# The first weights' products of two MLP layers by Strassen's seven half products, on one Trainium2 core

## The reference, cut to what matters

```python
# attention: x is (1152, 512)
h = np.maximum(x @ w_in, 0.0)                 # w_in 512 x 2048
x = h * h @ w_out                             # w_out 2048 x 512
p = domain_probs / (domain_probs.sum(-1, keepdims=True) + 1e-09)
for e in range(4):                            # w1[e] 512 x 1024, w2[e] 1024 x 512
    out += p[:, e:e + 1] * (np.maximum(x @ w1[e], 0.0) @ w2[e])
```

## Time and profile before

| | |
|---|---|
| device time, three runs | 663.77, 667.1, 667.3 us; median 667.1 |
| the profiled execution's own time | 664.17 us |
| its span | 662.4 us |
| mean granted PE clock | 0.997 of full |
| busy: PE, DVE, ACT, POOL | 641.6, 233.4, 152.7, 201.0 us |
| DMA | 35.51 MB, mean 54 GB/s |

### The profile page before, as it was taken

How to read it: one execution, slowest core, us unless ns; L and a number is a source line. 1 busy time by engine, 2 the same in 40 slices (tenths; PEclk the granted TensorE clock), 3 DMA queues, 4 the chain that set the end, 5 groups by cost and what they waited for, 6 DMA issues and landing times.

```text
span 662.4 us, 9433 instructions
## 1 busy us (share of the span) xinstructions
PE 641.6 (97%) x3684; PEld 601.5 (91%) x3684; DVE 233.4 (35%) x580; ACT 152.7 (23%) x377; POOL 201.0 (30%) x138
## 2 busy tenths in 40 slices
PE   6968999999999999999999999999999999999997
PEld 5858899999999999989898989898989898989896
DVE  5895945152956262312121212121212121212121
ACT  3776302031302031402031402031402031302020
POOL 4575725065915067500005500004500004500000
PEclk9999999999999999999999999999999999999999
DMA  8451300004310004310004210003300004010101
GB/s 323 162 172 62 96 33 0 1 1 128 94 34 1 1 0 128 97 33 0 1 1 127 95 32 0 0 0 127 95 32 0 0 0 127 0 48 0 48 0 48
DMA packets 16075, 35.51 MB, mean 54 GB/s; under 512 B 2480, under 2 KB 2736, under 8 KB 16048
## 3 DMA queue, kind: packets, MB, share of 16 engines
q1 hardware_dynamic: 16048, 35.15, 16.5%
HBM read 32.79 MB, written 2.36 MB: 53 GB/s over the span
## 4 chain that ended last, share of the span: by engine, by line
PE 91%; DVE 6%; DMA 1%; issue 1%; SPq 0%; POOL 0%; DVEq 0%; ACT 0%
PE ps L664 29%; PE ps L665 29%; PE ps L666 29%; DVE y_acc L460 1%; DVE probT_buf L485 1%; DMA raw<-in_moe_w_in 1%; PE ps L614 1%; PE ps L653 1%; PE ps L661 1%; DVE h_lo L509 1%; DVE h_hi L505 1%; PE ps L634 1%; DVE x_lo L491 0%; DVE wa_hi L498 0%; DVE ssum L476 0%
## 5 line engine op out<-in xcount | busy, mean ns | idle before, releaser
L664 PE MATMUL ps<-x_hi,wa_hi 128*128 128x384 f32 x576 | 193.2, 335 | 0.2 <-DVE h_lo L509 0.2
L666 PE MATMUL ps<-x_hi,wa_lo 128*128 128x384 f32 x576 | 192.6, 334 | 0.0
L665 PE MATMUL ps<-x_lo,wa_hi 128*128 128x384 f32 x576 | 192.5, 334 | 0.0
L442 ACT ACTIVATE h_hi<-ps 128x384 fp32r<-128x384 f32 x96 | 47.2, 492 | 318.8 <-PE ps L666 318.8
L313 POOL TENSOR_TENSOR wa_lo<-raw,wa_hi 128x1024 fp32r<-128x1024 f32 x24 | 57.1, 2404 | 202.9 <-ACT wa_hi L394 197.3
L666 PE MATMUL ps<-wb_hi,h_lo 128*128 128x512 f32 x288 | 112.3, 390 | 0.0
L665 PE MATMUL ps<-wb_lo,h_hi 128*128 128x512 f32 x288 | 112.3, 390 | 0.0
L664 PE MATMUL ps<-wb_hi,h_hi 128*128 128x512 f32 x288 | 112.0, 389 | 0.0
L664 PEld LDWEIGHTS ps<-x_hi,wa_hi 128*128 128x128 f32 x576 | 108.2, 188 | 1.1 <-DVE h_lo L509 0.5
L665 PEld LDWEIGHTS ps<-x_lo,wa_hi 128*128 128x128 f32 x576 | 108.2, 188 | 0.4
L666 PEld LDWEIGHTS ps<-x_hi,wa_lo 128*128 128x128 f32 x576 | 108.1, 188 | 0.0
(11 more groups left out here) (58 smaller groups left out, 494.3 us busy)
## 6 DMA issues: line engine op xcount, KB each, us to landing
raw<-in_moe_w SPq DMA_DIRECT2D x32, 512.0 KB, 3.6
raw<-in_moe_w_in SPq DMA_DIRECT2D x8, 512.0 KB, 5.1
raw<-in_moe_w_out SPq DMA_DIRECT2D x8, 512.0 KB, 4.2
out_acc<-in_q SPq DMA_DIRECT2D x8, 288.0 KB, 4.4
out_acc<-in_k SPq DMA_DIRECT2D x8, 288.0 KB, 4.4
result<-out_acc SPq DMA_DIRECT2D x8, 256.0 KB, 2.0
hid_tmp<-in_v_near SPq DMA_DIRECT2D x4, 384.0 KB, 4.5
v_str<-in_v_far SPq DMA_DIRECT2D x4, 320.0 KB, 6.1
```

The lines of the kernel that those rows point to most:

```text
L442: nc.scalar.activation(h_hi[:, ft, :], ps[:, ABANKS[ft % NB], 0:CH], ACT.Relu)\
L664: nc.tensor.matmul(dst, a_hi, b_hi, start=first, stop=False)
L665: nc.tensor.matmul(dst, a_hi, b_lo, start=False, stop=False)
L666: return nc.tensor.matmul(dst, a_lo, b_hi, start=False, stop=last)
```

## The change

The product of the first weights (`w_in`, `w1`) with the activations is no longer made tile by tile. Weights of a group of 512 features (k x f = 512 x 512) are cut into four quarters A11 to A22, the activations of a chunk of 576 tokens into four quarters B11 to B22 (halves of k, halves of 288 tokens). Seven products M1 to M7 of half size, of sums of quarters (S1 to S4, T1 to T4), and sums of these products (in Winograd's order: second, third, fourth sum, C11, C22, C21, C12) give the block's four quarters of hidden activations. The seven operand forms of each side are split into high and low as before. The parts:

- Groups of 512 features: 4 in the first layer and 2 for each of the 4 experts, 12 in all (`SUBS`), x 2 chunks of 576 tokens = 24 blocks `t`. PE's order is A0, A1, B0, A2, B1, ... A7, B6, B7, A8, A9, B8, ... (`A`: the seven products of a block, `B`: its outputs). All engines run it unrolled.
- Every product is 2 tiles (`u`) of 2 k-tiles x 3 passes of 288 columns. Products use banks in pairs: X (M1, M2, M4), Y (M6, M7, M3), Z (M5). Outputs use two banks in turn: in the first layer 8 tiles a block of 4 x 3 passes of 288 columns, in the experts 5 tiles for even and 4 for odd blocks, of 4 x 3 passes of 512 columns. An output tile waits for the DVE sum (`y_tile`, `out_tile`) of the tile two before.
- ACT copies M1 to SBUF (`first_product`), casts all forms (`wa_high`, `x_high`, `wb_high`) and hidden activations (`h_high`). POOL makes the low parts of all weight forms and x forms and the weights' sums S1 to S4 (`sums`; those of group 0 are DVE's), and no squares any more. DVE makes the T forms, all sums of products, the squares in place (`square`, one operation with ReLU), `h_low` from SBUF, and the outputs' sums.
- Attention's result goes to `y` (`att_out`, ACT), not to `x_hi` and `x_lo`; forms of chunk 0 are made in pairs 4 to 7 of the attention, those of chunk 1 behind it, those for the experts around B6, B7 and A8.
- Weights are laid out on the host in the order of the blocks; a group's first weights come as 4 DMAs of 256 KB, its second as 2 of 512 KB.

The core of the diff; `out_tile` is like `y_tile` with L592's operation on 512 columns. `t_forms` and `x_high` wait for the attention's or the first layer's results.

```diff
-    FT = F // P
-    CHUNKS = 3
-    CH = N // CHUNKS
-    TT = CH // P
-    PIECES = 4
-    NB = 4
-    UNITS = CHUNKS * FT
-    SPLIT_WITH = {0: [0, 1], 3: [2], 4: [3]}
+    GF = 512
+    FT = GF // P
+    MOE1_SUBS = 4
+    EXPERT_SUBS = 2
+    SUBS = MOE1_SUBS + EXPERTS * EXPERT_SUBS
+    CT = N // 2
+    HT = CT // 2
+    FORMS = 7
+    A11, S2, A12, S3, S1, A22, S4 = range(FORMS)
+    B11, T2, B21, T3, T1, T4, B22 = range(FORMS)
+    M1, M6, M2, M7, M5, M4, M3 = range(FORMS)
+    X, Y, Z = 2, 4, 0
+    PRODUCT_BANK = [X, Y, X, Y, Z, X, Y]
+    BBANK = 6
+    C11, C22, C21, C12 = range(4)
+    EVEN_TILES = 5
+    TILES = N // P
+
     LOCAL_CONSTANTS = 7
     CONSTANTS = LOCAL_CONSTANTS + 3
...
+        BLOCKS1 = 2 * MOE1_SUBS
+        ORDER = [("A", 0)]
+        for t in range(1, BLOCKS1):
+            ORDER += [("A", t), ("B", t - 1)]
+        ORDER += [("B", BLOCKS1 - 1), ("A", BLOCKS1)]
+        for t in range(BLOCKS1 + 1, 2 * SUBS):
+            ORDER += [("A", t), ("B", t - 1)]
+        ORDER += [("B", 2 * SUBS - 1)]
...
+            def wa_low(s, k):
+                where, i = {A11: (raw_a, 0), A12: (raw_a, 1), A22: (raw_a, 3),
+                            S1: (s_form, 0), S2: (s_form, 1), S3: (s_form, 2), S4: (s_form, 3)}[k]
+                pool.wait_ge(s_wa_hi, FORMS * s + k + 1)
+                nc.gpsimd.tensor_tensor(wa_lo[:, k, :, :], where[:, i, :, :], wa_hi[:, k, :, :].bitcast(F32),
+                                        ALU.subtract).then_inc(s_wa_lo, 1)
...
+            def sums(s):
+                pool.wait_ge(s_raw_a, 64 * (s + 1))
+                pool.wait_ge(s_wa_hi, FORMS * s)
+                pool.wait_ge(s_wa_lo, FORMS * s)
+                nc.gpsimd.tensor_tensor(s_form[:, 0, :, :], raw_a[:, 2, :, :], raw_a[:, 3, :, :], ALU.add)\
+                    .then_inc(s_s, 1)
+                nc.gpsimd.tensor_tensor(s_form[:, 2, :, :], raw_a[:, 0, :, :], raw_a[:, 2, :, :], ALU.subtract)\
+                    .then_inc(s_s, 1)
+                pool.wait_ge(s_s, 4 * s + 1)
+                nc.gpsimd.tensor_tensor(s_form[:, 1, :, :], s_form[:, 0, :, :], raw_a[:, 0, :, :], ALU.subtract)\
+                    .then_inc(s_s, 1)
+                pool.wait_ge(s_s, 4 * s + 3)
+                nc.gpsimd.tensor_tensor(s_form[:, 3, :, :], raw_a[:, 1, :, :], s_form[:, 1, :, :], ALU.subtract)\
+                    .then_inc(s_s, 1)
...
+            def x_low(i, k):
+                c = i % 2
+                pool.wait_ge(s_xf_hi, FORMS * i + k + 1)
+                if k == T2:
+                    pool.wait_ge(s_t, 4 * i + 3)
+                if i == 1 and k == 0:
+                    pool.wait_ge(s_pv, NP - 2)
+                src = x_blocks(c)[0].get(k, t_form[:, c, k, :, :])
+                nc.gpsimd.tensor_tensor(xf_lo[:, c, k, :, :], src, xf_hi[:, c, k, :, :].bitcast(F32),
+                                        ALU.subtract).then_inc(s_xf_lo, 1)
...
+            for k in range(FORMS):
+                x_low(1, k)
+            for kind, t in ORDER:
+                s = t // 2
+                if kind == "A" and t % 2 == 0 and s + 1 < SUBS:
+                    sums(s + 1)
+                if kind == "A" and t % 2 == 1:
+                    for d in range(KT):
+                        wb_low(s, d)
+                    if s + 1 < SUBS:
+                        for k in range(FORMS):
+                            wa_low(s + 1, k)
+                if kind == "B" and t in (BLOCKS1 - 2, BLOCKS1 - 1):
+                    for k in range(FORMS):
+                        x_low(t - BLOCKS1 + 4, k)
 
...
+            def first_product(t):
+                for u in range(2):
+                    act.wait_ge(s_m, products(t, M1, u))
+                    if t > 0:
+                        act.wait_ge(s_c, 8 * (t - 1) + u + 1)
+                    nc.scalar.activation(m1[:, u, :], ps[:, X + u, 0:HT], ACT.Copy).then_inc(s_m1, 1)
...
+            first_product(0)
+            att_out(NP - 2)
+            x_high(1, 0)
+            att_out(NP - 1)
+            h_high(0, C11)
+            for k in range(1, FORMS):
+                x_high(1, k)
+            for q in (C22, C21, C12):
+                h_high(0, q)
+            for kind, t in ORDER[1:]:
+                s = t // 2
+                if kind == "B":
+                    if t == BLOCKS1 - 2:
+                        for k in range(FORMS):
+                            x_high(2, k)
+                    continue
+                first_product(t)
+                if t % 2 == 1:
+                    wb_high(s, 0)
+                    wb_high(s, 1)
+                h_high(t, C11)
+                if t % 2 == 1:
+                    wb_high(s, 2)
+                    wb_high(s, 3)
+                if t == BLOCKS1:
+                    for k in range(FORMS):
+                        x_high(3, k)
+                for q in (C22, C21, C12):
+                    h_high(t, q)
+                if t % 2 == 1 and s + 1 < SUBS:
+                    for k in range(FORMS):
+                        wa_high(s + 1, k)
...
+            def second_sum(t):
+                for u in range(2):
+                    dve.wait_ge(s_m, products(t, M6, u))
+                    dve.wait_ge(s_m1, 2 * t + u + 1)
+                    nc.vector.tensor_tensor(u2[:, u, :], ps[:, Y + u, 0:HT], m1[:, u, :], ALU.add).then_inc(s_u, 1)
...
+            def c_block(t, q):
+                for u in range(2):
+                    if q == C11:
+                        dve.wait_ge(s_m, products(t, M2, u))
+                        bank, other = X, m1
+                    elif q == C22:
+                        dve.wait_ge(s_m, products(t, M5, u))
+                        dve.wait_ge(s_u, 6 * t + 2 + u + 1)
+                        bank, other = Z, u3
+                    elif q == C21:
+                        dve.wait_ge(s_m, products(t, M4, u))
+                        bank, other = X, u3
+                    else:
+                        dve.wait_ge(s_m, products(t, M3, u))
+                        dve.wait_ge(s_u, 6 * t + 4 + u + 1)
+                        bank, other = Y, u2
+                    nc.vector.tensor_tensor(cc[:, u, q, :], ps[:, bank + u, 0:HT], other[:, u, :], ALU.add)\
+                        .then_inc(s_c, 1)
+            def square(t, q):
+                for u in range(2):
+                    dve.wait_ge(s_c, 8 * t + 2 * q + u + 1)
+                    c = cc[:, u, q, :]
+                    nc.vector.scalar_tensor_tensor(out=c, in0=c, scalar=0.0, in1=c, op0=ALU.max, op1=ALU.mult)\
+                        .then_inc(s_sq, 1)
...
+            def rest_of_block(t):
+                c_block(t, C22)
+                fourth_sum(t)
+                if moe1(t):
+                    square(t, C22)
+                c_block(t, C21)
+                h_low(t, C22)
+                if moe1(t):
+                    square(t, C21)
+                c_block(t, C12)
+                h_low(t, C21)
+                if moe1(t):
+                    square(t, C12)
+                h_low(t, C12)
...
+            second_sum(0)
+            c_block(0, C11)
+            third_sum(0)
+            square(0, C11)
+            t_forms(1, T1, T2)
+            c_block(0, C22)
+            fourth_sum(0)
+            t_forms(1, T4, T3)
+            c_block(0, C21)
+            c_block(0, C12)
+            h_low(0, C11)
+            for q in (C22, C21, C12):
+                square(0, q)
+                h_low(0, q)
...
+            for kind, t in ORDER[1:]:
+                if kind == "A":
+                    second_sum(t)
+                    c_block(t, C11)
+                    if moe1(t):
+                        square(t, C11)
+                    if t == BLOCKS1:
+                        t_forms(3, T4)
+                    third_sum(t)
+                    if t == BLOCKS1:
+                        t_forms(3, T3)
+                    h_low(t, C11)
+                    rest_of_block(t)
+                elif moe1(t):
+                    for i in range(2 * KT):
+                        y_tile(t, i)
+                        if t == BLOCKS1 - 2 and i == KT - 1:
+                            t_forms(2, T1)
+                        if t == BLOCKS1 - 1 and i == 0:
+                            t_forms(2, T4)
+                        if t == BLOCKS1 - 1 and i == 1:
+                            t_forms(2, T3)
+                        if t == BLOCKS1 - 1 and i == KT - 1:
+                            t_forms(3, T1)
+                    if t >= BLOCKS1 - 2:
+                        t_forms(t - BLOCKS1 + 4, T2)
+                else:
...
+            def product(t, k):
+                s, c = divmod(t, 2)
+                if c == 0:
+                    pe.wait_ge(s_wa_hi, FORMS * s + k + 1)
+                    pe.wait_ge(s_wa_lo, FORMS * s + k + 1)
+                if x_set(t) is not None:
+                    pe.wait_ge(s_xf_hi, FORMS * x_set(t) + k + 1)
+                    pe.wait_ge(s_xf_lo, FORMS * x_set(t) + k + 1)
```

(117 more changed lines are left out.)

538 lines of the change are left out of this document (247 added, 291 removed).

## The result

The changed kernel takes **692.2 us** (median of four runs, 690.7 to 694.3) against 666.9 for the kernel before on the same chip (four runs, 663.8 to 667.3): ratio 1.039, 95% interval 1.035 to 1.044. It is slower. The forecast was 681 (640 to 698), slower with 0.56: the direction and the range held, the time was 11 us longer than forecast. The profiled run took 692.8 for a span of 691.0, so its sum is made against the 664.2 and 662.4 of before, 28.6 us apart.

A forecast was written before the change was run, and what follows sets the result against it. PE, 97% busy, was taken to bound the kernel by matmul count times spacing. 634 us without new waits, plus 24.8 steady, 12.9 start, 1.7 clock, 6 for A(8), A(9) and 2 experts, gave 681, range 640 to 698.

The forecast's parts named there:

- The matmuls, 29.2 us: TensorE's stream: 2784 matmuls of 288 columns 133 ns apart plus the experts' 196.7 us, 567.0 in all, 29.2 us less.
- I put the two together at 0, range -4 to +4: End of A(0) and the attention: DVE's saving of some 4 us and ACT's added casts net 0; A(0) ends at 72.3.
- Steady waits, 24.8: First-MLP output blocks B(0) to B(6): PE waits for DVE's y_tile, 4 x 2.9 plus 3 x 4.4 us, bounds 13 and 35.
- the two kinds: Stalls in first-MLP B blocks: 4.4 us with POOL's weight sums colliding, 2.9 with one wb_low collision.
- Start, 12.9: Before M2 of A(1): block 0's squares and h_low on DVE, with nine POOL collisions, cost 12.9 us, bounds 3.9 and 18.
- A(8), A(9), 6: Where the experts' second-chunk forms are made: DVE's collisions with POOL delay M6 and M7 of A(9), 6 us, bounds 0 and 9.
- Experts, 2: Seven even expert blocks: sums' collisions use up 1.9 us in hand and 0.3 more each, 2 us, bounds 0 and 12.
- At half speed that loses another 1.7: After the long start wait: the clock falls to the 1.2 GHz level for 3.4 us, losing 1.7 us.
- rival 4: Stalls of 4 us in every pair of blocks drop the clock each time, or x_low and wa_low lag: over 698; 9%.
- The port costing little (653): Rival 1: POOL's ops fall where DVE runs PSUM ops, so collisions cost little; 653 us, faster; 30%.
- That all hides: Rival 2: all the additions on DVE hide behind PE, giving 634 us; 6%.
- The weight load as pace: Rival 3: the weight load sets the matmuls' spacing at 288 columns, 173 ns, giving 745 us, slower; 3%.

## Why the prediction was right or wrong

- **The matmuls, 29.2 us:** right. 133.1 ns against 133, though the rows before had none of 288 columns. The Trainium skill, TensorE: Matmul & The Clock Gate, § "Wait — 56ns, not 53.3ns?", gives columns / 2.4 + 2.5 ns for back-to-back matmuls, from which an estimate for 288 is 122.5 ns. This kernel's matmuls, each with a weight load of its own, stand further apart, for 288 as for 512 columns (227.7 ns against the page's 215.7), so the sum was right to go by this kernel's own spacings.
- **"I put the two together at 0, range -4 to +4":** wrong, 5.7 us and outside the range. The step that failed was that two low halves ahead of pair 7's scaling delay it by their own length, to near 61.4, so that M7 ends at 64.4 and the values at 67.5. The last scaling began at 66.54 and ended near 66.8, M7 of A(0) ended near 70.4, and the values of pair 7 began at 71.93. I had priced what POOL does and left out what DVE and POOL hold up in each other (1.69 and 1.88 us on operations of 0.16) and the low clock in the attention; the rows put 2.0 us on the first and 2.6 on the second. The x forms ahead of the maximum, which I blamed next, were not it. No run tests the rest of this account.
- **Steady waits, 24.8:** measured 21.7. The places, the releaser and the two kinds were right: 2.9 forecast and 2.44 found; 4.4 forecast and 3.76, 3.22 and 3.82 found.
- **Start, 12.9:** 13.1 at M2 (and 1.1 at M1, where I had none). The mechanism is right too: the run without squares kept 10.9 of it, and the one without weight sums there 9.1. How close the number came may be partly luck: it was reckoned from an A(0) that ends at 72.3, and no run shows what the wait would be with A(0) on time.
- **A(8), A(9), 6:** measured 5.7. **Experts, 2:** measured 0, so the 1.9 us in hand were enough for the collisions.
- **"At half speed that loses another 1.7":** wrong by 9. I charged the low clock to the long wait alone and kept its repetition for rival 4. It came after waits of 2.4 us as well. (The low clock ahead of 78 us is part of the attention's 5.7.)
- **Rivals.** The port costing little (653) fell: POOL's weight sums moved away gave back 12 us, and even without squares the start kept its wait. That all hides fell with y_tile. The weight load as pace fell at 133 ns. Rival 4 came half true: the clock dropped often, and the time still stayed under 698. Of the 11 us of miss, 5.7 are the attention and 9.0 the clock, less 3.7 of waits that were smaller than forecast.
- **The shared port.** 1.05 us a collision, and DVE's eight h_low one per POOL operation, say it in this kernel's rows. The Trainium skill, SBUF — State Buffer, § SBUF: two separate sides, calls the shared pair an exclusive lock for a whole instruction; the trace agrees (0.82 against 2.93 us for two squares). In these rows a small DVE operation of 126 x 5 with a single SBUF operand, 0.16 us alone, waits out POOL's as well (1.69 us, and 2.22 in the kernel with the forms moved).

## What to carry to other kernels

When work moves from a full engine to ones that look half empty, write out each engine's queue in order for one period and find the operation that frees the next bank: here moving two y tiles from behind 26 operations a few places up gave back 17 us, the clock's share included. DVE operations with both operands in SBUF shouldn't stand beside POOL's; gate POOL's movable work to a stretch where DVE reads PSUM, and count a block of such DVE operations as one POOL operation each. What the profile names as the end of a wait is only the last link: ask what it stood behind before moving it.
